# Two chained expert layers after linear attention: the short tile transposed plainly, and three engines' phase loops written out

## The chip, the cores and the metric

The kernel runs on one core of a Trainium2 chip. The metric is the device time of one execution in microseconds (us), the median of several runs. TensorE is called PE, VectorE DVE, ScalarE ACT, GpSimd POOL, and SyncE SP.

## The reference, cut to what matters

Attention without softmax over 8 batches, 8 heads, 576 positions and 64 channels is followed by a first mixture of 8 experts (each token goes to the expert of its largest logit) and a second one with a capacity. The second one is the part that the change touches:

```python
def _moe2_ref(x, w_gate, w1, w2):
    N, D = x.shape            # 4608, 512
    E = w_gate.shape[1]       # 8 experts, w1 is 8 x 512 x 1024, w2 is 8 x 1024 x 512
    cap = N // E              # 576 tokens each
    logits = x @ w_gate
    # highest logits first: a token goes to the expert if it is free and has room
    ...
    for e in range(E):
        mask = assigned == e
        h = np.maximum(x[mask] @ w1[e], 0.0)
        out[mask] = h @ w2[e]
```

## The kernel before, in words

The attention and the routing, and the first expert layer (43 tiles of 128 rows, to about 792 us of the trace), are written out without loops on every engine. They are the same before and after, apart from one small DVE instruction.

The second expert layer fills its experts one after another. `select(kk, u)` on DVE finds which expert fills next and which tokens it takes: a threshold is searched digit by digit, in 19 steps. In each step DVE prepares an operand (`ask`), PE does a small f16 matmul on it (`search`: L871, L875, L881, L885, L888) and DVE takes the result up. DVE waits for that matmul before it goes on, and between asking and waiting it does other work that is due (`beside_step`: the low parts of weights and of activations, the token list).

An expert that is filled is computed in a phase: `phase(j, u)` on PE and on ACT. Its 576 tokens are 5 tiles, four of 128 rows and a last one of 64, the short tile (T2 = 5, LAST = 64). Values are split into a high and a low part. A full tile's product is a sum of three passes, high by high, high by low and low by high (L740). In the short tile the high rows stand in the upper half of the 128 rows and the low rows in the other half, so that one pass serves both (L758), and the two halves of the result must be added afterwards. The search matmuls of the experts to come are woven into the phase at fixed points of PE's program (`searches`, `POINTS`); a point is two large matmuls. So PE's order is written out by hand, and PE stops at a search matmul whose operand DVE has not made.

For a full tile, the hidden rows h (128 x 1024) are transposed by 8 PE transposes (L815) into two PSUM banks; ACT copies them to `hT_hi` (L1073) and DVE makes `hT_lo` (L1341). For the short tile `h_turned` multiplies by `fold` (128 x 64, two identities above each other; L813) in place of transposing, which adds the halves on the way; ACT then applies the relu (L1070) and DVE makes the low part beside it in `hT_hi` (L1337). The second product of a phase's short tile is done in the next phase, behind the first product of that phase's first tile. When DVE sees to its part of the short tile is fixed by the table `windows`, kind "h", g = 0.

The loops: DVE runs `select` 0 and 1 written out and selects 2 to 7 as three rounds of a loop (L1595). PE and ACT run phases 0, 1, 6 and 7 written out and phases 2 to 5 as two rounds. SP loads the weights of experts 0 and 1 written out and the others in three rounds (L524, 8 transfers of 512 KB each). In a loop, waits count against register values.

Of the kernel before, what the change touches and what calls it, by code (L numbers as in the profile page):

```python
# [30 lines left out]
P = 128  # L31
# [28 lines left out]
def build(nc, q, k, v, g_norm, w_gate, w_og, w1, w2, w_gate2, w21, w22, out, debug=None):  # L60
# [64 lines left out]
    windows = []  # L125
    for g in range(T2):
        follows = (FIRST_AT + [cycle])[g + 1]
        windows.append(("h", g, FIRST_AT[g] + 3, SECOND_AT[g] + (-1 if g == 0 else 7)))
        if g == 0:
            windows.append(("y", g, follows + 3, SECOND_AT[1] - 2))  # L130
        windows.append(("x", g, SECOND_AT[g] + 3, follows + (-1 if g == T2 - 2 else 3)))
# [14 lines left out]
    with ExitStack() as ctx:  # L146
# [22 lines left out]
        ident = sb("ident", [P, P])  # L169
        ones = sb("ones", [P, P])  # L170
        ones_h = sb("ones_h", [P, P], F16)
        fold = sb("fold", [P, LAST])
        own_group = sb("own_group", [GROUP * E, GROUP])
        own_expert = sb("own_expert", [GROUP * E, E])
        less_own = sb("less_own", [GROUP * E, E])
# [114 lines left out]
        s_made = sem("list_made")  # L290
        s_out = [sem(f"out_stored{i}") for i in range(2)]
        s_yu = sem("upper_y_copied")
        s_yg = [sem(f"y_rows_gathered{i}") for i in range(2)]
        s_whi = sem("weights_high")
        s_wlo = sem("weights_low")
# [78 lines left out]
        y2 = sb("y2", [P, DM])  # L374
        xst = [sb(f"xst{i}", [P, XW]) for i in range(3)]
        upper = xst[0][0:LAST, 0:DM]
        xgs = [xg, xg2]
        ys = [y, y2]
        ids = sb("ids", [P, T1, 2])
# [80 lines left out]
        def _(sp):  # L460
# [67 lines left out]
            sp.wait_ge(s_l2, T1 + 1)  # L528
            for kk in range(2):
                load_phase(kk, kk)  # L530
            with sp.Fori(1, E // 2) as j:
                for u in range(2):
                    kk = j * 2 + u
                    sp.wait_ge(s_l2, (kk - 1) * T2 + (T1 + 1))
                    alone(sp)
                    load_phase(kk, u)


        @block.gpsimd
# [116 lines left out]
        def _(pe):  # L656
# [148 lines left out]
                    mm = pe.transpose(tx_ps[:, c * P:c * P + rows], xgs[w % 2][0:rows, c:DM:KC], ident[0:rows, 0:rows])  # L805
                mm.then_inc(s_tx, 1)

            def h_turned(n, short=False):
                for half in range(2):
                    pe.wait_ge(s_h, n * 2 + 2)  # L810
                    for i in range(FC // 2):
                        if short:
                            mm = pe.matmul(th_ps[half][:, i * P:i * P + LAST], h[:, half * 4 + i:F:FC], fold[:, :], start=True, stop=True)  # L813
                            continue
                        mm = pe.transpose(th_ps[half][:, i * P:(i + 1) * P], h[:, half * 4 + i:F:FC], ident[:, :])  # L815
                    mm.then_inc(s_th, 1)

# [107 lines left out]
            def phase(j, u):  # L925

                kk = j * 2 + u
                fixed = isinstance(kk, int)
                w1_parts, w2_parts = ([split_w[2 * u + i][k] for i in range(2)] for k in range(2))
                w2_before = [split_w[2 * (1 - u) + i][1] for i in range(2)]  # L930
                for vv in range(T2):
                    n = kk * T2 + (T1 + vv)
                    short = vv == T2 - 1
                    if vv == 0:
                        pe.wait_ge(s_whi, kk * PIECES + PIECES // 2)
                    low = kk * PIECES + PIECES // 2 if vv == 0 else None
                    for half in range(2):
                        at = FIRST_AT[vv] + half * (SHORT if short else FULL)
                        first_in_parts(n, w1_parts, half, low if half == 0 else None, lambda i: searches(kk, at + i), short)
                    if vv < T2 - 1 or not fixed or kk < E - 1:  # L940
                        y_rows_in(j, u, vv + 1)
                    if vv > 0 or not fixed or kk > 0:
                        all_w = kk * PIECES + PIECES if vv == 1 else None
                        second_in_parts(n - 1, w2_before if vv == 0 else w2_parts, all_w, all_w,
                                        lambda i: searches(kk, SECOND_AT[vv] + i), vv == 0)
                    else:
                        for i in range(2 * SHORT):
                            searches(kk, SECOND_AT[vv] + i)
                    h_turned(n, short)

            for n in range(STEPS):
                search(0, n)
            for n in range(LISTED + 1):
                search_and_list(1, n)
            y_rows_in(0, 0, 0)
            phase(0, 0)
            phase(0, 1)
            with pe.Fori(1, E // 2 - 1) as j:
                for u in range(2):
                    phase(j, u)  # L960
            phase(E // 2 - 1, 0)
            phase(E // 2 - 1, 1)
            second_in_parts(NT2 + T1 - 1, [split_w[2 + i][1] for i in range(2)], None, None, lambda i: None, True)


# [1 line left out]
        def _(act):  # L967
# [95 lines left out]
                act.wait_ge(s_y, j * (2 * T2) + (T1 + w))  # L1063
                act.activation(upper, y_ps[LAST:2 * LAST, :], ACT.Copy).then_inc(s_yu, 1)

            def hT_high(n, short=False):
                for half in range(2):
                    act.wait_ge(s_th, n * 2 + (half + 1))
                    if short:
                        act.activation(hT_hi[:, half * 4:(half + 1) * 4, 0:LAST],  # L1070
                                       th_ps[half][:, :].rearrange("p (c t) -> p c t", t=P)[:, :, 0:LAST], ACT.Relu).then_inc(s_hT, 1)
                        continue
                    act.activation(hT_hi[:, half * 4:(half + 1) * 4, :].rearrange("p a b -> p (a b)"), th_ps[half][:, :],  # L1073
                                   ACT.Copy).then_inc(s_hT, 1)

            def weights_high(kk, u, pieces):
                for i in pieces:
# [4 lines left out]
            def phase(j, u):  # L1082
                kk = j * 2 + u
                fixed = isinstance(kk, int)
                for vv in range(T2):
                    n = kk * T2 + (T1 + vv)
                    short = vv == T2 - 1
                    relu(n, short)
                    if vv < T2 - 1 or not fixed or kk < E - 1:
                        rows_high(n + 1, vv == T2 - 2)  # L1090
                    if vv > 0:
                        y_copy(j, u, vv - 1)
                    elif not fixed or kk > 0:
                        upper_y(j - 1 + u, 1 - u)
                    hT_high(n, short)
                    if vv >= T2 - 3 and not (fixed and kk == E - 1):
                        weights_high(kk + 1, 1 - u, ((0, 1, 2), (3, 4, 5), (6, 7))[vv - (T2 - 3)])

# [15 lines left out]
            act.activation(h[:, 0:DM], tx_ps[:, :], ACT.Copy).then_inc(s_ytc, 1)  # L1114
            weights_high(0, 0, range(PIECES))
            rows_high(T1)
            phase(0, 0)
            phase(0, 1)
            with act.Fori(1, E // 2 - 1) as j:
                for u in range(2):  # L1120
                    phase(j, u)
            phase(E // 2 - 1, 0)
            phase(E // 2 - 1, 1)
            upper_y(E // 2 - 1, 1)


# [1 line left out]
        def _(dve):  # L1128
# [41 lines left out]
            for s in range(STEPS_A + 3):  # L1170
# [44 lines left out]

                if s == STEPS_A - 5:
                    blocks_of = ident[0:GROUP * E, 0:GROUP * E].rearrange("p (g e) -> p g e", e=E)
                    ch.inc(dve.tensor_tensor(fold[:, :], ident[:, 0:LAST], ident[:, LAST:2 * LAST], ALU.add))
                    ch.inc(dve.tensor_reduce(own_group[:, :], blocks_of, AX, ALU.add))
                    ch.inc(dve.tensor_reduce(own_expert[:, :], blocks_of.rearrange("p g e -> p e g"), AX, ALU.add))  # L1220

# [107 lines left out]
                dve.tensor_tensor(xT_lo[:, :, :].rearrange("p a b -> p (a b)"), tx_ps[:, :],  # L1329
                                  xT_hi[:, :, :].rearrange("p a b -> p (a b)").bitcast(F32), ALU.subtract).then_inc(s_xlo, 1)  # L1330

            def hT_low(n, short=False):
                for half in range(2):
                    dve.wait_ge(s_hT, n * 2 + (half + 1))
                    if short:
                        four = slice(half * 4, (half + 1) * 4)
                        dve.scalar_tensor_tensor(out=hT_hi[:, four, LAST:2 * LAST], in0=th_ps[half][:, :].rearrange("p (c t) -> p c t", t=P)[:, :, 0:LAST],  # L1337
                                                 scalar=0.0, in1=hT_hi[:, four, 0:LAST].bitcast(F32),
                                                 op0=ALU.max, op1=ALU.subtract).then_inc(s_hlo, 1)
                        continue  # L1340
                    dve.tensor_tensor(hT_lo[:, half * 4:(half + 1) * 4, :].rearrange("p a b -> p (a b)"), th_ps[half][:, :],  # L1341
                                      hT_hi[:, half * 4:(half + 1) * 4, :].rearrange("p a b -> p (a b)").bitcast(F32),
                                      ALU.subtract).then_inc(s_hlo, 1)

            def halves_added(kk, u):

# [81 lines left out]
            def duties(kk, u, n, table):  # L1428

                fixed = isinstance(kk, int)  # L1430
                for kind, g in table[n]:
                    tile = kk * T2 + g
                    if kind == "h" and not (fixed and tile == 0):
                        hT_low(T1 + tile - 1, g == 0)
                    elif kind == "x" and not (fixed and tile == NT2 - 1):
                        rows_low(T1 + tile + 1, g == T2 - 2)
                    elif kind == "y" and not (fixed and tile == 0):
# [150 lines left out]
                link(dve.tensor_tensor(score[:, :, :], score[:, :, :], over_g(t8), ALU.min))  # L1588
                beside_step(kk, u, BIDS)

            select(0, 0)
            start = ch.n + ch.base
            select(1, 1)
            per = ch.n + ch.base - start
            with dve.Fori(1, E // 2) as j:  # L1595
                ch.enter(j * (2 * per) + (start - per))
                for u in range(2):
                    select(j * 2 + u, u)
                assert ch.n == 2 * per, (ch.n, per)

            for n in range(EARLY):
                list_beside(E - 1, 1, n)
# [6 lines left out]
                    weights_low(E - 1, 1, i)  # L1609
            for n in range(EARLY):  # L1610
                duties(E - 1, 1, n, DUTIES)
            hT_low(T1 + NT2 - 1, True)
            halves_added(E - 1, 1)


# [23 lines left out]
```

## Time and the profile before

| | |
|---|---|
| Median of 3 runs | 1471.27 us (1468.60 to 1473.19) |
| The profiled execution | 1468.89 us |
| Its span, first to last instruction | 1467.1 us |
| Mean granted TensorE clock | 0.932 |
| Large instructions: PE 7648, DVE 2319, ACT 785, POOL 323 | 23013 instructions in the span |

Times in the rows are us from the span's start. PE is the matmul side and PEld the weight load. "issue" is time in which an engine waited for nothing that the profile shows. The start times of the short tiles' L813 matmuls serve as marks of the phases: 943.48 (phase 0), 1016.55, 1095.01, 1166.69, 1245.24, 1316.91, 1383.12 and about 1446.2 (phase 7).

### The profile page before, as it was taken

How to read it: one execution, taken by the hardware profiler on the slowest of the kernel's cores; microseconds unless marked ns; L12 is line 12 of the kernel's file. 1: busy time of each engine (PE TensorE's matmuls, PEld its weight loads, DVE VectorE, ACT ScalarE, POOL GpSimd, SP SyncE). 2: the span in 40 equal slices, each digit the busy share in tenths (PEclk: the TensorE clock that was granted, in tenths of full speed). 3: DMA queues.
4: the chain of work that ended last, by engine and by line, in shares of the span. 5: the costliest groups of instructions: out<-in, count | busy, mean ns of one | idle time of the engine just before them, and what ended most of it. 6: DMA issues, size and time to landing. Idle time of an engine off the chain costs nothing.

```text
span 1467.1 us, 23013 instructions
## 1 busy us (share of the span) xinstructions
PE 1297.8 (88%) x7648; PEld 1045.3 (71%) x7648; DVE 978.7 (67%) x2319; ACT 438.3 (30%) x785; POOL 387.7 (26%) x323
## 2 busy tenths in 40 slices
PE   5988816899999999999996249999899989999996
PEld 4877715788788888888885136777677767777885
DVE  1566595567677776777777787787678768776420
ACT  1655531222222222222221112323232423232421
POOL 1244334956533360751000010111111211111110
PEclk9989857999999999999998569999999999999998
DMA  9999126696514151451110313141414141413100
GB/s 217 246 253 314 58 69 221 199 384 227 157 45 143 60 159 48 154 152 44 39 36 23 114 30 126 44 137 44 137 44 137 45 137 37 144 44 136 44 29 18
DMA packets 70897, 172.18 MB, mean 117 GB/s; under 512 B 11624, under 2 KB 30136, under 8 KB 70144
## 3 DMA queue, kind: packets, MB, share of 16 engines
q1 hardware_dynamic: 46576, 108.61, 24.9%
q0 software_dynamic: 12112, 39.87, 8.5%
q10 hardware_dynamic: 12096, 22.19, 4.8%
q8 instruction: 71, 1.16, 0.4%
q14 instruction: 42, 0.34, 0.1%
HBM read 129.42 MB, written 41.23 MB: 116 GB/s over the span
## 4 chain that ended last, share of the span: by engine, by line
PE 72%; DVE 11%; DMA 6%; POOL 5%; issue 4%; ACT 1%; SPq 1%; POOLq 0%; DVEq 0%; ACTq 0%
PE bank L740 50%; PE bank L758 4%; PE bank L815 4%; POOL w_lo L577 3%; PE o_ps L702 2%; PE bank L871 2%; DMA xst<-x_rows,tok_i 2%; PE bank L813 2%; DMA x_sorted<-xst 1%; PE bank L805 1%; PE kv_ps L668 1%; DMA v_sb<-in_v 1%; POOL w_hi L575 1%; DVE xrow L1192 1%; PE qt_ps L690 1%
## 5 line engine op out<-in xcount | busy, mean ns | idle before, releaser
L1361 DVE SCALAR_TENSOR_TENSOR bank<-bank,factor,wg2b 128x512 f32<-128x512 f32 x336 | 254.7, 758 | 10.4
L1341 DVE TENSOR_TENSOR hT_lo<-bank,hT_hi 128x512 fp32r<-128x512 f32 x150 | 96.5, 685 | 171.6 <-ACT hT_hi L1073 169.9
L1026 ACT ACTIVATE h<-bank 128x512 f32<-128x512 f32 x166 | 99.2, 599 | 324.5 <-PE bank L740 320.7
L740 PE MATMUL bank<-w_hi,xT_hi 128*128 (+1 forms) x600 | 177.8, 419 | 6.2 <-POOL w_lo L577 2.6
L632 POOL DMA_INDIRECT xg<-y_rows,gat_i x40 | 40.5, 1012 | 530.5 <-DVE sca_i L1482 397.1
L740 PE MATMUL bank<-w_lo,xT_hi 128*128 (+1 forms) x600 | 176.6, 410 | 0.0
L740 PE MATMUL bank<-w_hi,xT_lo 128*128 (+1 forms) x600 | 169.5, 404 | 0.0
L740 PE MATMUL bank<-w_hi,hT_hi 128*128 (+1 forms) x600 | 160.5, 410 | 5.2 <-DVE score L1364 3.7
L740 PE MATMUL bank<-w_lo,hT_hi 128*128 (+1 forms) x600 | 159.2, 402 | 0.0
L740 PE MATMUL bank<-w_hi,hT_lo 128*128 (+1 forms) x600 | 155.7, 398 | 0.0
L577 POOL TENSOR_TENSOR w_lo<-w_sb,w_hi 128x1024 fp32r<-128x1024 f32 x56 | 134.3, 2399 | 4.5
L740 PEld LDWEIGHTS bank<-w_hi,xT_lo 128*128 128x128 f32 x600 | 114.7, 193 | 27.3
L740 PEld LDWEIGHTS bank<-w_lo,xT_hi 128*128 128x128 f32 x600 | 113.9, 193 | 26.9
L740 PEld LDWEIGHTS bank<-w_hi,hT_lo 128*128 128x128 f32 x600 | 111.8, 188 | 26.6
L740 PEld LDWEIGHTS bank<-w_lo,hT_hi 128*128 128x128 f32 x600 | 111.8, 190 | 25.8
L740 PEld LDWEIGHTS bank<-w_hi,hT_hi 128*128 128x128 f32 x600 | 109.6, 193 | 26.5 <-issue 5.6
L740 PEld LDWEIGHTS bank<-w_hi,xT_hi 128*128 128x128 f32 x600 | 108.6, 194 | 27.7 <-issue 7.9
L575 POOL CAST w_hi<-w_sb 128x1024 fp32r<-128x1024 f32 x56 | 58.4, 1043 | 178.8 <-DMA w_sb<-in_moe_w 178.7
L1033 ACT ACTIVATE y<-bank,factor 128x512 f32<-128x512 f32 x43 | 29.5, 687 | 224.7 <-PE bank L740 202.5
L639 POOL DMA_INDIRECT out<-y,sca_i x40 | 40.7, 1019 | 181.8 <-ACT y L1057 119.0
L1073 ACT ACTIVATE hT_hi<-bank 128x512 fp32r<-128x512 f32 x150 | 81.4, 597 | 24.6 <-PE bank L815 17.6
L585 POOL TENSOR_TENSOR xrow<-xrow,rin 96x512 f32<-96x512 f32 x48 | 54.5, 1166 | 122.6 <-DVE rin L1214 122.5
(258 smaller groups left out, 1891.9 us busy)
## 6 DMA issues: line engine op xcount, KB each, us to landing
w_sb<-in_moe_w SPq DMA_DIRECT2D x112, 512.0 KB, 6.2
y_rows<-y ACTq DMA_DIRECT2D x43, 256.0 KB, 2.9
x_sorted<-xst SPq DMA_DIRECT2D x41, 260.0 KB, 5.2
xg<-x_sorted ACTq DMA_DIRECT2D x41, 260.0 KB, 2.7
k_sb<-in_k SPq DMA_DIRECT2D x16, 576.0 KB, 15.2
v_sb<-in_v SPq DMA_DIRECT2D x16, 576.0 KB, 17.6
q_sb<-in_q SPq DMA_DIRECT2D x8, 1152.0 KB, 20.9
x_rows<-xrow POOLq DMA_DIRECT2D x16, 576.0 KB, 6.1
```

Of the source, the lines that this page charges most:

```text
L575: pool.tensor_copy(w_hi[:, 1 - e % 2, cols(i)], w_sb[:, e % 2, cols(i)]).then_inc(s_phi, 1)
L577: pool.tensor_tensor(w_lo[:, e % 2, cols(i)], w_sb[:, e % 2, cols(i)], w_hi[:, 1 - e % 2, cols(i)].bitcast(F32), ALU.subtract).then_inc(s_ ...
L585: pool.tensor_tensor(xv, xv, rin[b % 2][:, c * H:(c + 1) * H].unsqueeze(2).to_broadcast([PT, H, D]), ALU.mult).then_inc(s_xn, 1)
L632: pool.indirect_dma_start(out=xgs[w % 2][0:rows, 0:DM], out_offset=None, in_=y_rows[:, :], in_offset=bass.IndirectOffsetOnAxis(ap=gat_i[0: ...
L639: pool.indirect_dma_start(out=out[:, :], out_offset=bass.IndirectOffsetOnAxis(ap=sca_i[0:rows, w:w + 1], axis=0), in_=ys[w % 2][0:rows, :] ...
L740: mm = pe.matmul(ps, a[:, i % chunks, :], b[:, i % chunks, cols], start=(i == 0), stop=(i == 3 * chunks - 1))
L758: mm = pe.matmul(ps[0:rows, :], act[:, c, 0:rows], w[rows < P][:, c, cols], start=(i == 0), stop=(i == 2 * chunks - 1))
L815: mm = pe.transpose(th_ps[half][:, i * P:(i + 1) * P], h[:, half * 4 + i:F:FC], ident[:, :])
L1026: act.activation(h[:, half * HALF:(half + 1) * HALF], h_ps[half][:, :], ACT.Copy if short else ACT.Relu).then_inc(s_h, 1)
L1073: act.activation(hT_hi[:, half * 4:(half + 1) * 4, :].rearrange("p a b -> p (a b)"), th_ps[half][:, :], ACT.Copy).then_inc(s_hT, 1)
L1341: dve.tensor_tensor(hT_lo[:, half * 4:(half + 1) * 4, :].rearrange("p a b -> p (a b)"), th_ps[half][:, :], hT_hi[:, half * 4:(half + 1) * ...
L1361: ch.link(dve.scalar_tensor_tensor(out=prod_ps[:, :], in0=y1_ps[t % 2][:, :], scalar=factor[:, t:t + 1], in1=wg2b[:, e, :], op0=ALU.mult, ...
```

## The change

The short tile's h is transposed as a full tile is, by 8 transposes of 128 x 128. ACT copies the upper 64 columns of each group to SBUF (`sumT`, in a staging buffer that is free by then), DVE adds the lower ones, then makes the relu's high part with one instruction and the low part with another. In `windows` the due point of this DVE work moves from 3 to 2, so that it stands beside step 12 of a select (point 2 of a phase) and no longer beside step 13 (point 5). The matrix `fold` and its one DVE instruction go. The loops of DVE, PE, ACT and SP over experts are written out.

```diff
-        windows.append(("h", g, FIRST_AT[g] + 3, SECOND_AT[g] + (-1 if g == 0 else 7)))
+        windows.append(("h", g, FIRST_AT[g] + (2 if g == 0 else 3), SECOND_AT[g] + (-1 if g == 0 else 7)))
...
+        sumT = xst[1][:, 0:FC * LAST].rearrange("p (c t) -> p c t", t=LAST)
...
-            with sp.Fori(1, E // 2) as j:
-                for u in range(2):
-                    kk = j * 2 + u
-                    sp.wait_ge(s_l2, (kk - 1) * T2 + (T1 + 1))
-                    alone(sp)
-                    load_phase(kk, u)
+            for kk in range(2, E):
+                sp.wait_ge(s_l2, (kk - 1) * T2 + (T1 + 1))
+                load_phase(kk, kk % 2)
...
-                        if short:
-                            mm = pe.matmul(th_ps[half][:, i * P:i * P + LAST], h[:, half * 4 + i:F:FC], fold[:, :], start=True, stop=True)
-                            continue
                         mm = pe.transpose(th_ps[half][:, i * P:(i + 1) * P], h[:, half * 4 + i:F:FC], ident[:, :])
...
+            def upper_hT(n):
+                for half in range(2):
+                    act.wait_ge(s_th, n * 2 + (half + 1))
+                    act.activation(sumT[:, half * 4:(half + 1) * 4, :],
+                                   th_ps[half][:, :].rearrange("p (c t) -> p c t", t=P)[:, :, LAST:2 * LAST], ACT.Copy).then_inc(s_hTu, 1)
...
-            phase(0, 0)
-            phase(0, 1)
-            with pe.Fori(1, E // 2 - 1) as j:
-                for u in range(2):
-                    phase(j, u)
-            phase(E // 2 - 1, 0)
-            phase(E // 2 - 1, 1)
+            for kk in range(E):
+                phase(kk // 2, kk % 2)
...
+            def hT_short(n):
+                for half in range(2):
+                    t = th_ps[half][:, :].rearrange("p (c t) -> p c t", t=P)
+                    dve.wait_ge(s_hTu, (n - T1) // T2 * 2 + half + 1)
+                    ch.inc(dve.tensor_tensor(sumT[:, half * 4:(half + 1) * 4, :], t[:, :, 0:LAST], sumT[:, half * 4:(half + 1) * 4, :], ALU.add))
+                ch.wait()
+                dve.tensor_scalar(hT_hi[:, :, 0:LAST], sumT, 0.0, None, ALU.max).then_inc(s_hT, 2)
+                dve.wait_ge(s_hT, n * 2 + 2)
+                dve.scalar_tensor_tensor(out=hT_hi[:, :, LAST:2 * LAST], in0=sumT, scalar=0.0, in1=hT_hi[:, :, 0:LAST].bitcast(F32),
+                                         op0=ALU.max, op1=ALU.subtract).then_inc(s_hlo, 2)
...
-            with dve.Fori(1, E // 2) as j:
-                ch.enter(j * (2 * per) + (start - per))
-                for u in range(2):
-                    select(j * 2 + u, u)
+            for kk in range(E):
+                select(kk, kk % 2)
...
-            hT_low(T1 + NT2 - 1, True)
+            hT_short(T1 + NT2 - 1)
```

## Rows read from the trace of the kernel before

**Rows 1.** The page: PE's busy line, and the chain's shares by engine.

```profile
PE 1297.8 (88%) x7648; PEld 1045.3 (71%) x7648; DVE 978.7 (67%) x2319; ACT 438.3 (30%) x785; POOL 387.7 (26%) x323
...
PE 72%; DVE 11%; DMA 6%; POOL 5%; issue 4%; ACT 1%; SPq 1%; POOLq 0%; DVEq 0%; ACTq 0%
```

**Rows 2.** Windows, mark to mark: length, busy PE PEld DVE ACT POOL, clock, DMA.

```profile
943.48:1016.55 73.07, 73.07 (x447) 55.55 (x446) 55.86 (x143) 23.53 (x38) 10.10 (x10) 0.98 0.28 91
1016.55:1095.01 78.46, 74.41 (x447) 56.44 (x446) 55.56 (x143) 23.54 (x38) 9.67 (x10) 0.96 0.25 85
1095.01:1166.69 71.68, 71.68 (x447) 54.66 (x446) 55.86 (x143) 23.54 (x38) 11.61 (x10) 1.00 0.28 93
1166.69:1245.24 78.55, 74.56 (x447) 56.52 (x446) 55.55 (x143) 23.54 (x38) 9.66 (x10) 0.96 0.25 85
1245.24:1316.91 71.67, 71.67 (x447) 54.65 (x446) 55.84 (x143) 23.54 (x38) 10.02 (x10) 1.00 0.28 92
```

**Rows 3.** Waits of DVE over the span: total, times, longest.

```profile
DVE room L1383 <- issue: 12.3, 2, 6.2
```

**Rows 4.** The chain at DVE's first loop edge: start, length, what.

```profile
1042.05 6.60 issue
```

**Rows 5.** Around that edge: PE's timeline, then windows with clock and DMA share.

```profile
1053.04 0.70 PE L871 MATMUL bank<-cmp,bid 128*32 128x60 f16 x11 [4.05 <-DVE cmp L1379]
```

```profile
1046.00:1053.00 7.00, 2.99 (x14) 2.11 (x13) 4.02 (x11) 1.62 (x4) 1.01 (x1) 0.96 0.98 373
1053.00:1060.00 7.00, 6.96 (x29) 5.16 (x30) 4.87 (x17) 0.41 (x1) 0.00 (x0) 0.55 0.03 9
```

**Rows 6.** The chain at short tiles, and a full tile's transposes (L815).

```profile
1095.01 3.64 PE bank L813 x16
1098.65 1.44 PE bank L740 x6
...
1110.28 0.88 PE bank L815 x8
...
1166.69 3.64 PE bank L813 x16
```

**Rows 7.** The chain: after the short tiles of phases 0 and 6, and a usual 24.

```profile
943.48 3.69 PE bank L813 x16
947.17 2.67 PE bank L740 x6
...
1118.22 5.59 PE bank L740 x24
...
1386.75 7.21 PE bank L740 x24
```

**Rows 8.** Timelines of ACT, DVE and PE around phase 3's start, and the page's L1341.

```profile
1095.04 0.60 ACT L1057 ACTIVATE y<-bank 128x512 f32<-128x512 f32 x1 [5.95 <-PE bank L740]
1096.77 0.38 ACT L1070 ACTIVATE hT_hi<-bank 128x256 fp32r<-128x256 f32 x1 [1.13 <-PE bank L813]
```

```profile
1100.53 0.21 DVE L1536 TENSOR_TENSOR counts<-bank,own_group 32x60 f32<-32x60 f32 x1 [5.13 <-PE bank L871]
...
1101.06 0.33 DVE L1539 SCALAR_TENSOR_TENSOR dense<-count,room_n,own_expert 32x120 f16<-32x120 f32 x1
1101.53 0.76 DVE L1337 SCALAR_TENSOR_TENSOR hT_hi<-bank,hT_hi 128x256 fp32r<-128x256 f32 x2
```

```profile
1102.02 0.09 PEld L875 LDWEIGHTS bank<-dense,ones_h 32*128 32x128 f16 x1 [0.36 <-issue]
```

```profile
L1341 DVE TENSOR_TENSOR hT_lo<-bank,hT_hi 128x512 fp32r<-128x512 f32 x150 | 96.5, 685 | 171.6 <-ACT hT_hi L1073 169.9
```

**Rows 9.** The timeline of PE in the tail, last short tile's second product.

```profile
1451.03 0.47 PE L758 MATMUL bank<-w_hi,hT_hi 128*128 128x512 f32 x1 [1.02 <-DVE hT_hi L1337]
...
1454.33 2.21 PE L758 MATMUL bank<-w_hi,hT_hi 128*128 128x512 f32 x7
```

More of the change, by code:

```diff
@@ L171, in build @@
         ones_h = sb("ones_h", [P, P], F16)
-        fold = sb("fold", [P, LAST])
         own_group = sb("own_group", [GROUP * E, GROUP])
@@ L292, in build @@
         s_yu = sem("upper_y_copied")
+        s_hTu = sem("upper_hT_copied")
         s_yg = [sem(f"y_rows_gathered{i}") for i in range(2)]
@@ L806, in y_rows_in, with h_turned @@
                 mm.then_inc(s_tx, 1)
-            def h_turned(n, short=False):
+            def h_turned(n):
                 for half in range(2):
@@ L948, in phase @@
                             searches(kk, SECOND_AT[vv] + i)
-                    h_turned(n, short)
+                    h_turned(n)
             for n in range(STEPS):
@@ L1064, in upper_y, with hT_high @@
                 act.activation(upper, y_ps[LAST:2 * LAST, :], ACT.Copy).then_inc(s_yu, 1)
-            def hT_high(n, short=False):
+            def hT_high(n):
                 for half in range(2):
                     act.wait_ge(s_th, n * 2 + (half + 1))
[L1069 to L1072, printed above, removed]
                     act.activation(hT_hi[:, half * 4:(half + 1) * 4, :].rearrange("p a b -> p (a b)"), th_ps[half][:, :],
                                    ACT.Copy).then_inc(s_hT, 1)
+            def upper_hT(n):
[3 more added lines that the diff above has]
+                                   th_ps[half][:, :].rearrange("p (c t) -> p c t", t=P)[:, :, LAST:2 * LAST], ACT.Copy).then_inc(s_hTu, 1)
             def weights_high(kk, u, pieces):
@@ L1094, in phase @@
                         upper_y(j - 1 + u, 1 - u)
-                    hT_high(n, short)
+                    if short:
+                        upper_hT(n)
+                    else:
+                        hT_high(n)
                     if vv >= T2 - 3 and not (fixed and kk == E - 1):
@@ L1116, in _ @@
             rows_high(T1)
-            phase(0, 0)
-            phase(0, 1)
-            with act.Fori(1, E // 2 - 1) as j:
-                for u in range(2):
-                    phase(j, u)
-            phase(E // 2 - 1, 0)
-            phase(E // 2 - 1, 1)
+            for kk in range(E):
+                phase(kk // 2, kk % 2)
             upper_y(E // 2 - 1, 1)
@@ L1217, in _ @@
                     blocks_of = ident[0:GROUP * E, 0:GROUP * E].rearrange("p (g e) -> p g e", e=E)
-                    ch.inc(dve.tensor_tensor(fold[:, :], ident[:, 0:LAST], ident[:, LAST:2 * LAST], ALU.add))
                     ch.inc(dve.tensor_reduce(own_group[:, :], blocks_of, AX, ALU.add))
@@ L1330, in rows_low, with hT_low @@
                                   xT_hi[:, :, :].rearrange("p a b -> p (a b)").bitcast(F32), ALU.subtract).then_inc(s_xlo, 1)
-            def hT_low(n, short=False):
+            def hT_low(n):
                 for half in range(2):
                     dve.wait_ge(s_hT, n * 2 + (half + 1))
[L1335 to L1340, printed above, removed]
                     dve.tensor_tensor(hT_lo[:, half * 4:(half + 1) * 4, :].rearrange("p a b -> p (a b)"), th_ps[half][:, :],
@@ L1432, in duties @@
                     tile = kk * T2 + g
-                    if kind == "h" and not (fixed and tile == 0):
-                        hT_low(T1 + tile - 1, g == 0)
+                    if kind == "h" and g == 0 and not (fixed and tile == 0):
+                        hT_short(T1 + tile - 1)
+                    elif kind == "h" and not (fixed and tile == 0):
+                        hT_low(T1 + tile - 1)
                     elif kind == "x" and not (fixed and tile == NT2 - 1):
@@ L1589, in select @@
                 beside_step(kk, u, BIDS)
[L1591 to L1594, printed above, removed]
-            with dve.Fori(1, E // 2) as j:
-                ch.enter(j * (2 * per) + (start - per))
-                for u in range(2):
-                    select(j * 2 + u, u)
-                assert ch.n == 2 * per, (ch.n, per)
+            for kk in range(E):
+                select(kk, kk % 2)
             for n in range(EARLY):
```

## The prediction

> **What bounds the kernel now.** I read the page first. PE is busy for 88% of the span and holds 72% of the chain that ended last; DVE has 11% of that chain and "issue", waiting for nothing visible, 4% [rows 1]. The change lies almost wholly in the second expert layer, so the next view is the windows from one short tile's mark to the next [rows 2]. Each stretch holds the same work (447 matmuls on PE, 143 large instructions on DVE), yet they come in two lengths: 71.7 us in phases 3 and 5 (counting from the mark before), 78.5 us in the two others of the loop. In the short ones PE is busy for the whole stretch, DVE for 56 us of it: there PE's own work sets the pace, and what PE is spared is time saved. In the long ones PE has a hole of 4 us and is slow besides.
>
> The waits of DVE name the hole: two waits of 6.2 us each in front of the first instruction of a select (L1383), released by "issue" [rows 3]. The chain puts 6.60 us there, right behind the last instruction of select 3 [rows 4]; the second lies at 1192.3, behind select 5. Those are the two backward edges of DVE's loop (three rounds; L1595). PE meanwhile ran out of work that doesn't need the next select and stood for 4.05 us at its first search matmul [rows 5]. Then it ran at 0.55 of its clock for the 7 us behind, which is near the lower of its levels, 1.2 GHz, against 0.96 before and 1.00 in phase 3 [rows 2, 5].
>
> **The change part by part.** The sum is made against the profiled execution, 1468.9 us; the median of the three runs is 2.4 us above that.
>
> *DVE's edges go.* In a written-out program select 4 follows select 3 as select 5 follows select 4, and that seam costs nothing to be seen: no stretch with such a seam has a wait (phase 3 of rows 2). So the long stretches become short ones: 78.46 - 71.68 = 6.78 and 78.55 - 71.67 = 6.88, together **13.66 us**. Each is the 4.05 us hole plus some 2.8 us of slow clock. Bounds: 0 if the fetch of the code stalls all the same (a rival below), 13.7 if not. I take 13.7, because DVE's waits over the whole span show such a stall in these two places and nowhere else [rows 3], though all of the attention and of the first expert layer is written out.
>
> Here the Trainium skill, "Runtime: NRT & Kernel Launch", section "Instruction fetch mechanics", has the mechanism: fetch is sequential, a page ahead, and a taken branch to code outside the two pages held stalls on a DMA. The trace agrees with it for DVE, with 6.2 us per edge [rows 3]; it has no price of its own for the sum.
>
> *PE's, ACT's and SP's edges go.* PE's one backward edge lies behind the short tile of phase 3. The chain gives those 16 records 3.64 us there, just what it gives them in phase 2, where there is no edge [rows 6]. So the gain is 0; ACT's edge lies in the same place, before work that PE waits for only microseconds later, and is 0 too. SP's edges can at most delay the weights of the next expert, which nobody waits for in these stretches: PE is busy throughout [rows 2]. The register instructions and the idle semaphore increments before waits go as well; PE is full in looped stretches as in written-out ones, so again 0.
>
> *The short tile's transposes.* The multiplication by `fold` takes 3.64 us of PE per short tile [rows 6] (3.69 once, [rows 7]), and a full tile's 8 transposes 0.88 us. These are the operation that comes in its place, in the same banks and on the same h, so no bound is needed but the row. Seven short tiles stand where PE is the pace (phases 0 to 6): 3.69 + 6 x 3.64 - 7 x 0.88 = **19.4 us**. The eighth is in the tail.
>
> *The clock behind them.* Behind the short tiles of phases 0 and 6 the same matmuls take longer than usual: 6 in 2.67 us against 1.44, and 24 in 7.21 against 5.59 [rows 6, 7]. PE had no hole there; what it had run just before was the 16 records of `fold`. Behind the transposes of full tiles I see no such thing: phase 3's stretch holds four such groups at a clock of 1.00 [rows 2]. So these two dips, 1.23 + 1.62 = **2.9 us**, should go with `fold`. Bounds 0 and 2.9; two dips in seven is thin evidence, but the stretches where they occur are those with the odd load, and I take 2.9.
>
> *DVE's new work, and its place.* Call S the end of the transposes, when PE starts the next phase. Today DVE takes up step 12's result 1.88 us behind S (1100.53 against 1098.65), after 5.13 us of idleness, and has `dense` ready at 1101.39; PE loads it at 1102.02, so there are 0.63 us to spare [rows 6, 8]. After: ACT's copy of y starts with the transposes and takes 0.60 [rows 8], so to S - 0.25. The two copies to `sumT`, 128 x 256 at 0.38 as L1070's [rows 8], end at about S + 0.13 and S + 0.51. DVE's two additions cost as L1337's pair, 0.76: to about S + 0.9. A relu of 128 x 512 from SBUF isn't in the trace; it costs between one 128 x 256 half (0.38) and the 0.69 of a two-operand instruction of that size out of PSUM [L1341 in rows 8]. I take 0.69, as the size is the same. The low part is another 0.69. DVE is free at S + 2.0 to S + 2.3, up to 0.4 us later than the result comes, against 0.63 to spare; also the pair that stood in step 13 is gone. The work is about 1.4 us more per phase than before, covered by DVE's 5.13 us of idleness, of which the shorter transposition on PE takes 2.76. So **0**. If the cover is gone, because these estimates are 0.5 us too low, each of seven phases loses 0.3 us: 2 us. What is queued behind hT_short on DVE is step 12's take-up, and PE's search point 5 waits for that. The second product of the short tile waits for the new low part, but it stands some 7 us behind S: no wait.
>
> *The tail.* Today the last `fold` group takes its 3.64 us and PE then idles 1.02 before the second product [rows 6, 9]: 4.7 us. After: 0.88 of transposes, then the same chain as above, 2.0 to 2.3 us, and some 0.1 us to PE: 3.0 to 3.3. Gain 1.4 to 1.7; I take **1.4**. The 16 matmuls behind it take 5.51 us now (to 1456.54), at a low clock; PE idles longer in front of them after the change, so I leave them as slow.
>
> Sum: 13.7 + 19.4 + 2.9 + 0 + 1.4 = 37.4, so a profiled execution of 1431.5. The runs of before lay up to 4.3 us above the profiled one, in the median 2.4. I predict 1433 us for the median.
>
> **The rivals.**
>
> *The fetch stalls anyway (10%).* The DVE stall falls into a stretch in which the weights' transfers hold the DMA engines at 98% [rows 5]; PE's edge, at a quiet time, cost nothing. So perhaps it isn't the branch but a fetch that stands in line behind 4 MB of weights. Then a page border close behind the start of a load would stall too. Against it: phases 1, 3 and 5 have the same loads, and no stall. If one or both of the two stay: 1433 + 6.8 = 1440, or 1447.
>
> *DVE becomes late (10%).* The step-12 work ends later than I reckon, because ACT's copies are held up or the strided relu is dear. If it ends 1.5 us later in each of seven phases, PE loses 1.3 us in each and may lose clock: 1433 + 9 = 1442. The point from which it counts is S + 2.5.
>
> *The clock falls behind transposes (5%).* Transposes in place of matmuls leave PE doing less that counts as work. If each of seven short tiles got a dip like phase 6's, 1.6 us: 1433 + 2.9 + 11 = 1447. The Trainium skill, "TensorE: Matmul & The Clock Gate", "Part 4: PE-mode transpose", says that a transpose doesn't count as PE-busy in the usual way. The trace speaks against an effect at this length, with 1.00 over a stretch with four groups of them [rows 2, 6].
>
> *Slower than before (3%).* Written-out code must be fetched from memory for all eight selects and phases. If every page of DVE's code that falls under the weights' load stalled as the edges do, 6.8 us each, it would take 37.4 / 6.8, so six exposed pages in the seven phases, to end at or above 1469. In all written-out stretches of before there is not one.
>
> *More gain (7%).* The tail's clock holds, worth 5.51 - 3.84 (16 matmuls at the rate of rows 6, 1.44 for 6) = 1.7 us, and other brief dips around the early phases go: 1429.
>
> **How the numbers follow.** My own case has 65%, and its range is 1429 to 1437 (the clock term 0 to 2.9, the tail, the 4.6 us by which runs of before differ). The rivals on the slow side that still gain have 25%, most of it at 1438 to 1446. The range 1428 to 1443 leaves out about 2 in 10. Within 0.3% (4.4 us) is what a measurement of this kernel cannot tell from no change. All cases but the slow one, and the far end of the others, lie well below 1467: faster 0.96, same 0.01, slower 0.03.
>
> **What would show it.** No DVE wait on "issue" of over 1 us, and no 4 us wait of PE for L1379 behind phase 1. All stretches of rows 2 at about 68.9 us (71.7 less 2.76), with PE busy throughout and a clock of 1.00. L815 with 664 records, 64 more. The 6 matmuls behind the short tiles of all phases at 1.44 us. DVE's relu at 0.4 to 0.7 us, its take-up of step 12 at S + 1.9 to S + 2.3, and no PE wait before L875. The prediction is wrong if stretches stay at two lengths, if PE waits for `dense` or if the dips stay or multiply.

## The result

| | before | changed |
|---|---|---|
| Median | 1471.55 us (4 runs, 1468.60 to 1473.19) | 1431.13 us (4 runs, 1429.30 to 1434.31) |
| Ratio | | 0.973, 95% interval 0.9706 to 0.9754 |
| The profiled execution, its span | 1468.89, 1467.1 us | 1430.42, 1428.7 us |
| Mean granted TensorE clock | 0.932 | 0.941 |

The kernel became 40 us faster. 1433 was predicted (1428 to 1443), with the profiled execution at 1431.5; it is at 1430.4.

The page after, in the lines that answer to [rows 1]:

```profile
PE 1261.0 (88%) x7584; PEld 1011.1 (71%) x7584; DVE 985.4 (69%) x2334; ACT 437.6 (31%) x785; POOL 386.7 (27%) x323
```

PE has 37 us less to do and is the bound as before. The stretches from one short tile's transposition to the next say where the time went. These are the windows of the changed kernel, in the columns of [rows 2]:

```profile
942.64:1011.53 68.89, 68.89 (x440) 51.78 (x439) 56.85 (x145) 23.44 (x38) 9.89 (x10) 1.00 0.28 96
1011.53:1080.38 68.85, 68.85 (x440) 51.77 (x439) 56.63 (x145) 23.44 (x38) 9.70 (x10) 1.00 0.28 96
1080.38:1149.27 68.89, 68.89 (x440) 51.77 (x439) 56.86 (x145) 23.45 (x38) 10.42 (x10) 1.00 0.29 96
1149.27:1218.12 68.85, 68.85 (x440) 51.75 (x439) 56.88 (x145) 23.45 (x38) 9.89 (x10) 1.00 0.28 96
1218.12:1287.01 68.89, 68.89 (x440) 51.78 (x439) 56.87 (x145) 23.45 (x38) 9.89 (x10) 1.00 0.28 96
```

All five are 68.9 us, PE is busy through each, and its clock stands at 1.00; before they were 73.07, 78.46, 71.68, 78.55 and 71.67. No wait of DVE is released by "issue" any longer. The next thing to see is one short tile, in the timeline of the changed kernel behind phase 1. ACT's two copies to `sumT` are named xst here, by the buffer that holds them:

```profile
1011.37 1.05 PE L810 MATMUL bank<-ident,h 128*128 128x128 f32 x8
...
1012.07 0.78 ACT L1066 ACTIVATE xst<-bank 128x256 f32<-128x256 f32 x2
...
1012.48 0.82 DVE L1336 TENSOR_TENSOR xst<-bank,xst 128x256 f32<-128x256 f32 x2 [0.54 <-ACT xst L1066]
...
1013.41 0.43 DVE L1338 TENSOR_SCALAR hT_hi<-xst 128x512 fp32r<-128x512 f32 x1
...
1013.94 0.69 DVE L1340 SCALAR_TENSOR_TENSOR hT_hi<-xst,hT_hi 128x512 fp32r<-128x512 f32 x1
...
1014.54 0.20 DVE L1536 TENSOR_TENSOR counts<-bank,own_group 32x60 f32<-32x60 f32 x1
...
1015.74 0.09 PEld L870 LDWEIGHTS bank<-dense,ones_h 32*128 32x128 f16 x1 [0.36 <-DVE dense L1539]
```

With S at 1012.42, DVE takes up step 12 at S + 2.12, without having been idle before it, and `dense` is ready at 1015.39. PE loads it 0.35 us later, after the same 0.36 us gap as before [rows 8]. The releaser that is named there is DVE, so little is left to spare, but PE's chain doesn't become longer.

The tail, in PE's timeline, answers to [rows 9]:

```profile
1412.61 0.47 PE L756 MATMUL bank<-w_hi,hT_hi 128*128 128x512 f32 x1 [2.40 <-DVE hT_hi L1340]
...
1415.85 2.26 PE L756 MATMUL bank<-w_hi,hT_hi 128*128 128x512 f32 x7
```

PE idles 2.40 us where it idled 1.02, and its last 16 matmuls still take 5.50 us.

### The profile page after: what moved, and what is told of

Read it like the earlier page. It is cut to its first block, busy times and chain, and to the rows that moved or that the text cites. A ratio compares the mean times of both kernels' runs of the same rounds, so it can differ in the third digit from the quotient of the medians.

```text
span 1428.7 us, 21805 instructions
## 1 busy us (share of the span) xinstructions
PE 1261.0 (88%) x7584; PEld 1011.1 (71%) x7584; DVE 985.4 (69%) x2334; ACT 437.6 (31%) x785; POOL 386.7 (27%) x323
## 4 chain that ended last, share of the span: by engine, by line
PE 71%; DVE 9%; DMA 7%; POOL 6%; issue 4%; ACT 1%; SPq 1%; POOLq 0%; ACTq 0%; DVEq 0%
PE bank L738 52%; PE bank L810 4%; PE bank L756 4%; POOL w_lo L575 3%; DMA xst<-x_rows,tok_i 2%; PE bank L866 2%; PE o_ps L700 2%; DMA x_sorted<-xst 2%; PE bank L803 2%; DMA v_sb<-in_v 1%; POOL xrow L583 1%; POOL w_hi L573 1%; PE bank L793 1%; DMA w_sb<-in_moe_w 1%; PE kv_ps L666 1%
## 5 line engine op out<-in xcount | busy, mean ns | idle before, releaser
L738 PE MATMUL bank<-w_hi,xT_hi 128*128 (+1 forms) x600 | 175.9, 415 | 11.5 <-POOL w_lo L575 8.3
L738 PE MATMUL bank<-w_lo,xT_hi 128*128 (+1 forms) x600 | 174.4, 406 | 0.0
L738 PE MATMUL bank<-w_hi,xT_lo 128*128 (+1 forms) x600 | 167.9, 401 | 0.0
L738 PE MATMUL bank<-w_hi,hT_hi 128*128 (+1 forms) x600 | 159.8, 408 | 4.8 <-DVE score L1362 3.3
L738 PE MATMUL bank<-w_lo,hT_hi 128*128 (+1 forms) x600 | 158.6, 401 | 0.0
L738 PE MATMUL bank<-w_hi,hT_lo 128*128 (+1 forms) x600 | 155.7, 398 | 0.0
L738 PEld LDWEIGHTS bank<-w_hi,xT_lo 128*128 128x128 f32 x600 | 113.3, 191 | 26.9
L738 PEld LDWEIGHTS bank<-w_lo,xT_hi 128*128 128x128 f32 x600 | 112.6, 191 | 26.6
L738 PEld LDWEIGHTS bank<-w_hi,xT_hi 128*128 128x128 f32 x600 | 107.6, 192 | 32.8 <-issue 12.8
L738 PEld LDWEIGHTS bank<-w_hi,hT_lo 128*128 128x128 f32 x600 | 111.7, 188 | 26.7
L738 PEld LDWEIGHTS bank<-w_lo,hT_hi 128*128 128x128 f32 x600 | 111.3, 189 | 25.7
L738 PEld LDWEIGHTS bank<-w_hi,hT_hi 128*128 128x128 f32 x600 | 109.0, 192 | 26.0 <-issue 5.2
L810 PEld LDWEIGHTS bank<-ident,h 128*128 128x128 f32 x664 | 86.4, 190 | 7.6 <-ACT h L1016 0.4
L1059 ACT ACTIVATE hT_hi<-bank 128x512 fp32r<-128x512 f32 x150 | 81.4, 597 | 23.7 <-PE bank L810 17.2
```

Source lines behind the costliest of these rows:

```text
L738: mm = pe.matmul(ps, a[:, i % chunks, :], b[:, i % chunks, cols], start=(i == 0), stop=(i == 3 * chunks - 1))
```

## The experiments

The stages ahead of the second expert layer are the same in every kernel here, yet they end up to 8 us apart from one execution to another (the first short tile begins between 942.6 and 950.4 us). That moves whole runs, so beside the medians I give the time from the first short tile's transposition (phase 0) to the end of the span. It is 523.6 us before (1467.1 - 943.48) and 486.1 changed (1428.7 - 942.64). Of the 38.4 us between the spans, 0.8 lie ahead of that mark and are not the change's. The time from the mark comes from one profiled execution of each kernel; the changed kernel once more gave 486.0:

> The changed kernel unaltered, as the measure for the three beside it: 1431 us, from phase 0's short tile to the end 486 us.

Its median was 1432.36 us, the ratio to before 0.9748 (0.9724 to 0.9772), and its mark stood at 944.56 in a span of 1430.6.

**The two halves apart.** The loops of the kernel before written out, the short tile left as it was:

```diff
-            with dve.Fori(1, E // 2) as j:
...
+            for kk in range(E):
+                select(kk, kk % 2)
```

The loops of PE, ACT and SP went in the same way.

> The kernel before with all loops over experts written out and the short tile left with its multiplication by fold. My theory: DVE's two edges cost 13.7 us and fold the rest, so 1471.5 - 13.7 = 1458 us; the stretches between short tiles' marks become 71.7 us each, and the slow matmuls behind fold (the dips of clock behind phases 0 and 6) still occur in some phases, because fold is still there. Rival, the stall is not the branch's but that of a fetch under the weights' load: one or more DVE waits on issue of over 1 us stay, and the time is 1464 to 1471. Rival, the dips had nothing to do with fold: none here, 1455.

It gave 1454.86 us (8 runs, 1446.41 to 1463.27; ratio 0.9889, 0.9857 to 0.9921), and 511.2 us from the mark: 12.4 less than before. No wait at a select's start is left. The windows of this kernel behind phases 0, 1 and 2, and its chain behind phase 1's short tile:

```profile
944.03:1017.22 73.19, 73.19 (x448) 55.61 (x446) 55.62 (x143) 23.55 (x38) 9.88 (x10) 0.98 0.27 90
1017.22:1090.07 72.85, 72.85 (x447) 55.38 (x446) 55.38 (x143) 23.55 (x38) 9.71 (x10) 0.98 0.27 91
1090.07:1161.74 71.67, 71.67 (x448) 54.62 (x446) 55.40 (x143) 23.55 (x38) 9.88 (x10) 1.00 0.27 92
```

```profile
1017.22 3.69 PE bank L810 x16
1020.90 2.60 PE bank L737 x6
```

(L810 is the multiplication by `fold` here, L737 the large matmul.) The two edges' 13.7 us are won, and one more dip of the clock than before, behind three of the seven short tiles in place of two, takes 1.2 us back. So the dips stay where `fold` stays. The median fell on 1455, the number of the rival without dips, but its runs lie 17 us apart, and the trace shows the dips: the rival falls. Whether the third dip has to do with the loops or differs from one execution to the next, one trace doesn't tell.

The other half alone: the new short tile, with all four loops kept.

> The kernel before with the short tile's new transposes and DVE work alone, all four loops kept. My theory: 19.4 of PE, 2.9 of clock and 1.4 in the tail, so 1471.5 - 23.7 = 1448 us, stretches of 68.9 and 75.7 us, and both DVE waits on issue of about 6 us. Rival, the transposes hide a loss that the loops' removal made up for: above 1452.

It gave 1447.72 us (4 runs, 1443.97 to 1451.08; ratio 0.9844, 0.9808 to 0.9881) and 500.0 us from the mark, 23.6 less than before. The waits of DVE, and the windows behind phases 0, 1 and 3; the second holds DVE's first edge, the third its second edge and PE's:

```profile
DVE room L1394 <- issue: 12.4, 2, 6.2
```

```profile
944.83:1013.73 68.90, 68.90 (x440) 51.79 (x439) 56.72 (x145) 23.43 (x38) 9.96 (x10) 1.00 0.28 96
1013.73:1088.18 74.45, 70.43 (x439) 52.71 (x439) 56.85 (x145) 23.43 (x38) 9.69 (x10) 0.98 0.26 89
1157.10:1234.22 77.12, 71.55 (x439) 53.45 (x439) 56.64 (x145) 23.36 (x38) 9.66 (x10) 0.96 0.26 86
```

The two halves, 12.4 and 23.6, make 36.0 of the 37.5 us together. The next pair helps to tell what is missing.

**Which engine's loop.** DVE's loop alone put back into the changed kernel, and then the three others alone:

```diff
-            for kk in range(E):
-                select(kk, kk % 2)
+            with dve.Fori(1, E // 2) as j:
+                ...
+                for u in range(2):
+                    select(j * 2 + u, u)
```

> The changed kernel with DVE's loop alone put back (PE, ACT and SP written out). My theory: DVE's edges are all that the loops cost, so 13.7 us above the changed kernel: 1445 us, two waits on issue of about 6.2 us, each followed by a hole of some 4 us on PE and matmuls at the lower clock. Rival, the cost came from several engines' edges together: less than 10 us above.

> The changed kernel with the loops of PE, ACT and SP put back and DVE written out. My theory: no difference, 1431 us within 1.5 us, all stretches 68.9 us. Rival, that those edges and register waits cost too: 1434 or more, with a hole on PE at the start of phase 4.

DVE's loop gave 1445.04 us (4 runs, 1439.75 to 1449.70; ratio 0.9812, 0.977 to 0.9854), and 497.8 us from the mark: 11.7 more than the changed kernel, in two stretches of 75.76 and 73.71 us against 68.9. The waits on "issue" are 5.6 and 5.5 us. The rival of several engines together (less than 10 us) falls, but the price of an edge isn't fixed: the same two cost 13.7 us in the kernel before.

The other loops gave 1434.24 us (4 runs, 1433.03 to 1435.93; ratio 0.9755, 0.9725 to 0.9785), and 487.5 us from the mark, 1.4 more. So the rival was right in this: there is a hole, at the place of PE's edge, at the start of phase 4. The chain of that kernel (L813 is the transposes), then what ACT and PE do there:

```profile
1150.43 0.89 PE bank L813 x8
1151.31 1.17 issue
1152.48 1.66 PE bank L741 x6
```

```profile
1151.63 2.00 ACT L1081 ACTIVATE w_hi<-w_sb 128x1024 fp32r<-128x1024 f32 x2
1152.48 1.19 PE L741 MATMUL bank<-w_hi,xT_hi 128*128 128x512 f32 x4 [1.17 <-issue]
```

The run puts back three loops at once, but the hole is not ACT's: L1081 is the last work of ACT ahead of its own edge and ends at 1153.63, when PE is at work again. SP only starts transfers, whose weights PE gets by way of ACT and DVE. So PE's own edge is left. As I read it, that edge takes some 2 us, its 1.17 and the 0.89 that ran meanwhile. The 3.64 us of `fold` matmuls in PE's queue hid it [rows 6], and 0.89 us of transposes don't. With the new short tile in loops PE waits there too: in the half above, 1.4 us between the transposes and the next matmul (the profile names ACT's L1081 as releaser there, but the weights that PE waits for at that place were made earlier). Writing out PE's loop is thus worth nothing before and 1.4 us with the new short tile.

The 1.5 us that the two halves lack have three parts. The half without loops lacks 1.3 us (12.4 against 13.7), nearly all of it its third dip. In the half with loops PE's edge takes 1.4 us, but DVE's first edge costs 5.6 us (74.45 against 68.85) where it cost 6.8 before, which gives 1.2 back; the second costs 6.8 as before (77.12 - 68.85 - 1.45).

**Why DVE's edge costs 6 us.** SP's weight transfers start right ahead of the edge. Here they are held until DVE is over it, in the kernel with DVE's loop:

```diff
                 sp.wait_ge(s_exp, kk + 1)
+                if 2 <= kk < E - 1:
+                    sp.wait_ge(s_sel, (kk + 1) * STEPS + 1)
```

> The changed kernel with DVE's loop put back, and SP holding each expert's weight transfers until DVE has asked step 0 of the select behind, so that no transfers run while DVE goes over its loop's edge. If the 6 us stall is mostly a fetch standing in line behind 4 MB of weights, the wait on issue falls to 3 us or less and PE's hole to 1 us or less. If it is the branch's own fetch, it stays at 5 to 6 us, PE's hole at 4, and the time at 1445.

It gave 1437.52 us (4 runs, 1434.11 to 1442.26; ratio 0.9769, 0.9743 to 0.9795) and 488.9 us from the mark, against 497.8 with the transfers in their place. DVE's waits, then PE's timeline at the first edge, then the windows of the stall with the transfers in place (the kernel above, first row) and held back (second):

```profile
DVE room L1383 <- issue: 4.7, 2, 2.4
```

```profile
1046.17 0.48 PE L868 MATMUL bank<-cmp,bid 128*32 128x60 f16 x11 [0.20 <-DVE cmp L1379]
...
1049.34 0.22 PE L872 MATMUL bank<-dense,ones_h 32*128 32x120 f16 x1 [1.09 <-DVE dense L1541]
```

```profile
1042.00:1048.00 6.00, 6.00 (x31) 5.01 (x30) 0.38 (x2) 1.57 (x3) 1.02 (x1) 1.00 1.02 365
```

```profile
1039.00:1042.00 3.00, 3.00 (x15) 2.40 (x14) 0.61 (x2) 0.00 (x0) 0.00 (x0) 1.00 0.05 16
```

The stall is 2.3 to 2.4 us with the DMA engines at 0.05 and 5.5 to 6.2 with them full. The transfers of one queue of the DMA engines, which the profile calls instruction, show the difference. These are its rows in windows of 0.2 us, 1045.60:1045.80 with the transfers in place and 1040.00:1040.20 with them held back:

```profile
q14 instruction: 1, 0.01, 13.0%
```

```profile
q14 instruction: 1, 0.01, 17.7%
```

It is the only packet of its kind inside either stall. With quiet DMA engines it comes 0.4 to 0.6 us after DVE's last instruction (which ends at 1039.57), beside the weights 3.4 to 3.6 us after it (1042.24). From the packet to DVE's next instruction it is about as long in both, 1.8 to 2.3 us. The second edges look the same, with 0.3 to 0.5 and 3.3 to 3.5 us. So both theories hold a part: a fetch that the branch needs, of 2.3 us, and over 3 us in which it stands in line behind the weights. (The trace doesn't name the engine that a packet is for; that it is DVE's is read from its place.) The price on PE falls from about 6 to 1.4 us an edge, because its holes at the first edge shrink from 3.4 and 0.6 us to 0.2 and 1.1, and PE's clock doesn't fall behind them (1.00 in the 7 us from 1050).

**Is it `fold` that the clock falls behind?** First `fold` issued twice, in the kernel before with its loops written out, then the transposes of the changed kernel issued four times, which makes them about as long as `fold` was:

```diff
-                    for i in range(FC // 2):
+                    for i in [x for x in range(FC // 2) for _ in range(2 if short else 1)]:
```

> The kernel before with its loops written out, and each multiplication by fold issued twice (the same result; 7.3 us per short tile in place of 3.64). My theory: the clock falls because of a long stretch of fold's 64-column matmuls, so behind nearly every short tile the next matmuls are slow, in place of 3 of 7 places. Rival: the dips are not fold's doing, then 3 or fewer places. In time 29 us more for the doubled work, and 1.3 to 2 us for each further dip.

> The changed kernel with each of the short tile's transposes issued four times (the same result; 3.55 us in place of 0.89, about the length that fold had). My theory from the traces: transposes of this length leave the clock alone, so 21 us more than the changed kernel and all stretches at 71.55 us. Rival, that of a transposition that doesn't count as work for the clock: dips behind the short tiles as fold had them, or more, so 1.3 us or more on top in some stretches.

One execution of each: 1498.3 us and 548.4 from the mark, and 1459.38 us and 507.2 from the mark. The chains of the two, behind phase 3's short tile (L737 and L738 are the large matmuls):

```profile
1178.78 7.49 PE bank L810 x32
1186.27 2.67 PE bank L737 x6
```

```profile
1164.95 3.56 PE bank L810 x32
1168.51 1.39 PE bank L738 x6
```

With `fold` twice the next matmuls are slow behind all seven short tiles: 37.2 us more than with `fold` once, of which the doubled products are 30.8 (8 x 3.85), so 6.4 us go to more and deeper dips. With four times the transposes they are slow behind none, and the time is 486.0 + 8 x 2.67 = 507.4, as measured.

The granted clock shows where it falls. The first two windows are from the kernel before, the last 0.67 us of phase 0's `fold` and the matmuls behind it; the third is the end of the doubled `fold` above, the fourth the four times issued transposes above:

```profile
946.50:947.17 0.67, 0.67 (x4) 0.67 (x5) 0.00 (x0) 0.00 (x0) 0.00 (x0) 0.62 0.15 55
947.17:949.84 2.67, 2.67 (x8) 1.63 (x9) 0.00 (x0) 2.27 (x3) 0.00 (x0) 0.50 0.00 0
```

```profile
1184.00:1186.27 2.27, 2.27 (x11) 2.27 (x11) 0.00 (x0) 0.00 (x0) 0.00 (x0) 0.50 0.00 0
```

```profile
1164.95:1168.51 3.56, 3.56 (x34) 3.56 (x33) 0.99 (x2) 0.98 (x2) 0.99 (x1) 1.00 0.21 78
```

So here the clock falls to its lower level while `fold` still runs, and PE is busy throughout. (Behind phase 6 of the kernel before it falls right at `fold`'s end: 1.00 up to 1386.75, 0.59 in the 1.25 us behind.) `fold` itself is hardly slower for it (7.49 us for 32 records, 3.64 for 16); the 512-column matmuls behind pay. The dips are `fold`'s, and not those of a transposition. That its narrow products are the reason is my reading: `fold` differs from the four times issued transposes in the operation too, and puts 16 products of 64 columns through in the time of 32 of 128. No run tells these apart.

The Trainium skill, "TensorE: Matmul & The Clock Gate", "Part 4: PE-mode transpose", says that a transpose doesn't count as PE-busy the same way; at this length, 3.56 us, the granted clock stayed at 1.00 and shows nothing of that.

**The place of DVE's new work.** The due point put back to 3, beside step 13:

```diff
-        windows.append(("h", g, FIRST_AT[g] + (2 if g == 0 else 3), SECOND_AT[g] + (-1 if g == 0 else 7)))
+        windows.append(("h", g, FIRST_AT[g] + 3, SECOND_AT[g] + (-1 if g == 0 else 7)))
```

> The changed kernel with the due point of the short tile's DVE work at 3 as before, so that it stands beside step 13 and not step 12. My theory: step 13's take-up waits for some 2 us more of DVE work there, but PE's next search point lies some 7 us on, so no difference in time, within 1 us. Rival, that place lies on the path: PE waits for a compare of DVE in each of six phases, 3 us or more.

1434.61 us (4 runs, 1429.54 to 1439.62; ratio 0.9747, 0.9717 to 0.9776), and 487.6 from the mark, 1.6 more. I had expected at most 1. The chain shows the seam: DVE's work stands in it now, up to the compare that PE's next search matmul waits for.

```profile
1019.48 0.69 DVE hT_hi L1340
1020.17 1.14 DVE w_lo L1423
...
1022.18 0.84 DVE cmp L1377
...
1023.07 0.48 PE bank L866 x11
```

From one group of transposes to the next are 12.68 us in place of 12.48: 0.2 us per phase. Step 12 has idle time ahead of it (2.32 us in this kernel), step 13 has the low weights beside it.

**A version that is a little faster.** PE's hole in the tail filled:

```diff
+            for i in range(10):
+                pe.matmul(h_ps[0][:, :], xT_hi[:, i % KC, :], split_w[2][0][:, i % KC, 0:HALF], start=True, stop=True)
             second_in_parts(NT2 + T1 - 1, [split_w[2 + i][1] for i in range(2)], None, None, lambda i: None, True)
```

> The changed kernel with 10 matmuls of 512 columns whose result nobody reads, put on PE between the last short tile's transposes and its second product, where PE stands idle for 2.4 us. My theory: the low clock of the last 16 matmuls comes from that hole; with it filled they take 3.8 us and not 5.5, so 1.7 us less than the changed kernel. Rival, the clock falls anyway, because it answers to what PE did before: no difference, or up to 0.2 us more where the filling overlaps.

1431.04 us (5 runs; ratio 0.9732, 0.9715 to 0.9749) beside the changed kernel's 1432.36 on the same chip, and 484.5 us from the mark against 486.0. The medians' intervals overlap; the gain is read from the traces, one of each. PE's timeline in the tail of this kernel (L954 is the filling):

```profile
1411.93 2.58 PE L954 MATMUL bank<-w_hi,xT_hi 128*128 128x512 f32 x10
1414.58 0.47 PE L756 MATMUL bank<-w_hi,hT_hi 128*128 128x512 f32 x1
1414.88 2.00 PE L756 MATMUL bank<-w_lo,hT_hi 128*64 128x512 f32 x8
1416.73 1.79 PE L756 MATMUL bank<-w_hi,hT_hi 128*128 128x512 f32 x7
```

The last 16 matmuls take 3.94 us in place of 5.50, at a granted clock of 1.00 in place of 0.69. That is 1.56 us, a little under the 1.7 expected. So in the changed kernel's tail it is the hole that costs the clock.

## Why the prediction was right, point by point

The median is 1.9 us under the forecast; 1.1 of that is in the profiled execution, and 0.8 of these lie ahead of the second expert layer.

- *DVE's edges, 13.66 us.* The two long stretches shortened by 9.61 and 9.70 us, of which 2.79 each are the transposes': 13.7 us. With DVE's loop put back it was 11.7 us. The mechanism was half told: I took the stall as the branch's, and named the full DMA engines as a rival. They are about half of it, 3 of 6 us; no part of it came back in written-out code.
- *PE's edge, 0.* Right for the sum, since the kernel before shows no hole there. The reason given was that the edge costs nothing; as far as the runs show, it was hidden under `fold`, and it costs 1.4 us where only the short tile is changed. In that sense the two halves of the change need each other.
- *The transposes, 19.4 us.* 3.64 became 0.89 on the chain, and the stretches without an edge or a dip shortened by 2.79 each (71.68 to 68.89): 7 x 2.79 = 19.5.
- *The dips, 2.9 us.* The stretch behind phase 0 shortened by 4.18 and that behind phase 6 by 4.35 (63.26 to 58.91, from the short tile to the end of the last full product), so 1.39 and 1.56 beside the transposes: 2.95. The cause was argued from two cases of seven; the doubled `fold` and the four times issued transposes show it.
- *DVE's new work, 0.* The take-up came at S + 2.12, within S + 2.0 to 2.3. The relu took 0.43 us, near the lower end of its bounds, where I had taken 0.69; the additions took 0.82 and not 0.76, and DVE began a little before S + 0.13.
- *The tail, 1.4 us.* From the end of the last full product to the end of the span are 20.72 us before (1467.1 - 1446.38) and 19.36 after (1428.7 - 1409.34): 1.36. The clock in the tail stayed low, as was assumed.

The sum of the terms is 37.5 us, and the other 0.8 of the profiled difference lie ahead of the second expert layer, where no term was put.

My reading of the waits in written-out code holds, though a first look at the other traces speaks against it. I argued that such code never shows a stall of DVE on "issue". In the profiled executions of before and after there is none, nor in four others, but in the remaining six of the twelve the view of waits names "issue" in written-out code too, most of the time between 230 and 370 us: 11.2 us in four waits in the short tile's half, 9.4 in five in the kernel with DVE's loop, 15.0 in four with `fold` twice. One of these, in the timeline of ACT and DVE of the kernel with DVE's loop:

```profile
296.81 0.60 ACT L1059 ACTIVATE hT_hi<-bank 128x512 fp32r<-128x512 f32 x1 [2.34 <-remote]
...
297.44 0.69 DVE L1325 TENSOR_TENSOR hT_lo<-bank,hT_hi 128x512 fp32r<-128x512 f32 x1 [2.25 <-issue]
```

DVE needs what L1059 makes, and starts 0.03 us after its end. It is so in each of these waits, those of some 0.5 us in the second expert layer too: DVE goes on 0.02 to 0.11 us after the copy of ACT that it needs. They are ordinary waits for ACT, as the same lines have them elsewhere, and the view only misses the releaser. At the loop's edges no copy of ACT ends within 1 us ahead of L1383, so those two stalls are real. The rival of stalls in written-out code has thus no case in any of the twelve traces.

## What to carry to other kernels

Look for equal pieces of work that take unequal times, mark to mark: the difference of two such stretches priced the loop edges within 0.1 us of what before and after then showed, before anything was changed. But it is the price in that kernel and at that load: the same edges cost 11.7 and 12.4 us in others. As these runs read, a loop's edge costs what its engine's queue doesn't hide, and more when it falls beside a burst of transfers; a change that empties the queue brings the edge into view. Where PE must wait or do products like `fold`'s, the matmuls behind pay for it too, so count them with it. And look a wait on "issue" up in the timeline before calling it a stall: here some ended with another engine's work.

## What the runs showed of the hardware that was not expected

- A taken loop edge of DVE stalled 2.3 to 2.4 us with quiet DMA engines and 5.5 to 6.2 us beside 4 MB of transfers. A packet of the DMA queue named instruction came 0.3 to 0.6 us into the short stalls and 3.3 to 3.6 us into those of 5.5 and 5.6 us. One edge of PE, with 0.89 us of transposes ahead of it, left it idle for 1.2 us (1.4 in another kernel).
- 3.64 us of matmuls with 64 columns, back to back and without a hole, brought PE's granted clock to the lower level (0.50) in 2 or 3 of 7 cases, and 7.5 us of them in 7 of 7. In 3.56 us of back-to-back 128-column transposes it stayed at 1.00 in all 7.
- DVE's one-input relu of 128 x 512 from SBUF took 0.43 us, the two-input instruction of the same size 0.69. That is in line with the Trainium skill, "VectorE: DVE Perf Modes", "Mode 2×_2P — use both read ports for one tensor": one fp32 tensor without a second one is read through both ports.
